# Chunked linear attention ahead of two feed-forward stages: gate logits put before the transposes that turn a unit's rows back, and a weight piece split between two evacuations

## The reference, cut to what matters

```python
# 1: attention with a decaying state, per batch b and head h
state = gamma[h] * state + outer(k[t], v[t])
y[t]  = scale * q[t] @ state                    # x = y as 3072 rows of 512

# 2: each row goes to the one expert with the highest gate logit
logits = x @ w_gate                             # 8 experts
e_idx  = argmax(logits, axis=1)
h      = max(x[mask] @ w1[e], 0)                # 512 -> 1024
out[mask] = gate_w * sigmoid(x @ w_output_gate)[e] * (h @ w2[e])   # 1024 -> 512

# 3: rms norm, then a gated feed-forward layer of width 1536
out = (silu(xn @ w_gate2) * (xn @ w_val)) @ w_out
```

## Time and profile before

| | before |
|---|---|
| time, median of 3 runs | 1107.06 us (1105.83 to 1107.13) |
| the profiled execution's own time | 1104.48 us |
| its span in the profile | 1102.7 us |
| attention stage, from the q transposes of unit 1 to unit 23's `turn_x` | 12.69 to 136.92 us |
| TensorE busy | 1088.8 us (99%) |
| VectorE busy | 442.5 us (40%) |
| ScalarE busy | 378.7 us (34%) |
| GpSimd busy | 177.7 us (16%) |

### The profile page before, as it was taken

The page is one execution under the profiler, slowest core; times in us unless marked ns, Lnnn a source line. Parts: engine busy times, 40 slices in busy tenths (PEclk is TensorE's granted clock), DMA queues, the critical chain, the costliest instruction groups (busy, mean ns, idle before and its releaser), DMA issues.

```text
span 1102.7 us, 20452 instructions
## 1 busy us (share of the span) xinstructions
PE 1088.8 (99%) x6307; PEld 907.5 (82%) x6308; DVE 442.5 (40%) x886; ACT 378.7 (34%) x619; POOL 177.7 (16%) x245
## 2 busy tenths in 40 slices
PE   7999999999999999999999999999999999999998
PEld 6888887888888888887888888888888888888887
DVE  4777766342514425432433323423333243333222
ACT  3555534343525445433224231331133132213112
POOL 2444414222211211000010300210030011001000
PEclk9999999999999999999999999999999999999999
DMA  9999816333435434432101210111021001101001
GB/s 216 254 264 256 232 59 229 123 124 114 124 114 190 164 114 144 155 88 83 58 10 29 77 34 5 38 38 38 0 76 24 14 28 48 38 0 39 1 1 39
DMA packets 114069, 101.53 MB, mean 92 GB/s; under 512 B 81856, under 2 KB 87392, under 8 KB 114016
## 3 DMA queue, kind: packets, MB, share of 16 engines
q1 hardware_dynamic: 98752, 66.07, 22.1%
q0 software_dynamic: 8832, 26.81, 7.7%
q10 hardware_dynamic: 6432, 7.96, 2.1%
HBM read 76.41 MB, written 20.22 MB: 88 GB/s over the span
## 4 chain that ended last, share of the span: by engine, by line
PE 97%; issue 1%; DMA 1%; ACT 0%; POOL 0%; DVE 0%; SPq 0%; POOLq 0%
PE bank L730 15%; PE bank L731 15%; PE bank L732 15%; PE banks L654 14%; PE bank L627 14%; PE banks L730 3%; PE banks L731 3%; PE banks L732 3%; PE bank L538 2%; PE banks L524 2%; PE bank L568 2%; PE bank L576 1%; PE banks L642 1%; PE bank L618 1%; PE banks L517 1%
## 5 line engine op out<-in xcount | busy, mean ns | idle before, releaser
L1409 DVE TENSOR_TENSOR gated<-bank,sig 128x512 f32<-128x512 f32 (+1 forms) x78 | 50.7, 650 | 340.1 <-ACT sig L1022 337.1
L1022 ACT ACTIVATE sig<-bank 128x512 f32<-128x512 f32 x72 | 43.1, 598 | 325.4 <-PE bank L732 315.8
L730 PE MATMUL bank<-xh,w1h 128*128 128x512 f32 x384 | 149.4, 389 | 0.0
L731 PE MATMUL bank<-xl,w1h 128*128 128x512 f32 x384 | 149.4, 389 | 0.0
L732 PE MATMUL bank<-xh,w1l 128*128 128x512 f32 x384 | 149.4, 389 | 0.0
L1031 ACT ACTIVATE hh<-prod 128x512 fp32r<-128x512 f32 (+1 forms) x78 | 46.7, 599 | 109.9 <-DVE prod L1417 105.9
L730 PEld LDWEIGHTS bank<-xh,w1h 128*128 128x128 f32 x384 | 72.1, 188 | 15.0
L732 PEld LDWEIGHTS bank<-xh,w1l 128*128 128x128 f32 x384 | 72.1, 188 | 15.0
L731 PEld LDWEIGHTS bank<-xl,w1h 128*128 128x128 f32 x384 | 72.1, 188 | 14.9
L1176 DVE TENSOR_TENSOR hidl<-bank,hidh 128x512 fp32r<-128x512 f32 x29 | 20.1, 692 | 130.3 <-ACT hidh L881 130.3
L1423 DVE TENSOR_TENSOR hl<-prod,hh 128x512 fp32r<-128x512 f32 (+1 forms) x78 | 50.9, 652 | 51.2 <-ACT hh L1031 48.4
(11 more groups left out here) (243 smaller groups left out, 2139.5 us busy)
## 6 DMA issues: line engine op xcount, KB each, us to landing
stage<-in_moe_w SPq DMA_DIRECT2D x64, 512.0 KB
expert_rows<-tile_o ACTq DMA_DIRECT2D x29, 256.0 KB
q_raw<-in_q SPq DMA_DIRECT2D x24, 256.0 KB
k_raw<-in_k SPq DMA_DIRECT2D x24, 256.0 KB
v_raw<-in_v SPq DMA_DIRECT2D x24, 256.0 KB, 5.0
stage<-stage SPq DMA_DIRECT2D x64, 64.0 KB, 2.0
stage<-in_moe_w_out SPq DMA_DIRECT2D x6, 512.0 KB
stage<-in_moe_w_gate SPq DMA_DIRECT2D x5, 512.0 KB
```

Of the source, the lines that this page charges most:

```text
L730: pe.matmul(out_ap, lh, rh, start=first, stop=False)
L731: pe.matmul(out_ap, lh, rl, start=False, stop=False)
L1022: nc.scalar.activation(sig[:], bank[GV[f % 2][0]][:, :], ACT.Sigmoid).then_inc(s["sig_done"], 1)
L1409: v3.tensor_tensor(gated[:, part], bank[GV[f % 2][0]][:, part], sig[:, part], ALU.mult)\
```

## The change

In TensorE's step `gate_logits(u - 1)` now stands ahead of `turn_x(u - 1)`. In ScalarE's step the split of a weight piece now stands between `evacuate_yT(u - 1)` and `evacuate_x(u - 1)`.

```diff
@@ TensorE, step(u)
                 scores(u)
                 if u:
+                    gate_logits(u - 1)
                     turn_x(u - 1)
-                    gate_logits(u - 1)
@@ ScalarE, step(u)
                 evacuate_turned(u)
                 if u:
                     evacuate_yT(u - 1)
-                    evacuate_x(u - 1)
                 for i in range(PRE_A):
                     if piece_step(i) + 2 == u:
                         split_hi(i % PER, (w1h, w2h)[i // PER % 2], i // RUN * HALF + (i % PER) * PIECE, i // STAGE + 1)
+                if u:
+                    evacuate_x(u - 1)
```

## The result

| | before | after |
|---|---|---|
| median of the runs | 1107.10 us (1105.83 to 1107.26, 4 runs) | 1116.64 us (1115.89 to 1119.04, 4 runs) |
| ratio to before, 95% interval | | 1.0092 [1.0075, 1.0110] |
| the profiled execution's own time | 1104.48 us | 1115.89 us |
| its span | 1102.7 us | 1114.1 us |
| opening of unit 1 to opening of unit 23 | 16.68 to 136.92: 120.24 us | 16.20 to 148.28: 132.08 us |

The change made the kernel 0.92% slower, 9.5 us between the medians and 11.4 us between the two profiled executions. The "opening" of a unit is T of the prediction, where the weight loads behind the scores begin.

A forecast was written before the change was run, and what follows sets the result against it. TensorE, busy for 99% of the span, was taken as the bound. Losses of 10.0 (20 units), 0.40 (unit 12) and 0.88 us (unit 22) sum to 11.3, added to the median 1107.06 for 1118.4 us; range 1115.0 to 1121.7.

The forecast's parts named there:

- The bank wait, 20 x 0.50: K transposes wait for the x_out copy to free turn_x's bank: 0.50 us in each of 20 units, 10.0 us.
- the row behind the last step: Trace row with logits already first; copy started 1.71 us after their first load, giving a loss of 0.65 per unit.
- end of the copy + 0.05 - 1.71: Loss of a unit in us, if positive, from the x_out copy's end counted from T; k loads start undisturbed at 1.67.
- The exchange itself, costed at nothing: TensorE's turn_x, logits and q transposes (0.39, 0.81, 0.47 us) only change places; the exchange by itself adds zero.
- Unit 12 and unit 22: Exceptions: unit 12 loses 0.40, having already lost 0.10 to a late scatter; unit 22 0.88, its logits waiting for slot indices.
- The sum: Whole loss in the attention stage: 10.0 + 0.40 + 0.88 = 11.3 us, giving 1118.4 us.
- The piece: Weight split on ScalarE between the evacuations: 1.05 us, covered by idle time before the copy; no cost.
- The hidden wait: Rival: the k transposes' bank wait stays hidden, the copy ending by T + 1.66; no change, 1107.1 us; chance 0.03.
- the gain from fewer changes of shape: Rival: logits follow the scores without the 0.12 us gap in 23 units, 2.8 us faster, 1104.3; chance 0.02.
- No piece was late: Answers a rival: weight pieces landing late hold the copy back in 12 units, adding 8.0 us, 1126.4; chance 0.06.
- The clock stayed at 1.00: Answers a rival: the clock falls in the run of 12 transposes, adding 26 us, 1144.8; chance 0.02.

The follow-up runs named there:

- own_bank: Changed kernel with turn_x writing unused halves of the outputs' two banks; the outputs, not the k transposes, wait for the x_out copy: 1109.45 us, ratio 1.0025.
- q_ahead: Changed kernel with the next unit's q transposes moved between the logits and turn_x, so the k transposes directly follow turn_x: 1128.22 us, ratio 1.0188.
- q_ahead_old_order: Kernel before with the next unit's q transposes moved ahead of turn_x, leaving only the logits between turn_x and the k transposes: 1113.39 us, ratio 1.0067.
- own_bank_wait_last: Same as own_bank, but the outputs' wait for the x_out copy stands last among their waits, behind that for the state: 1108.08 us, ratio 1.0013.
- three_buffers: Kernel before with a third x_out buffer, so a copy waits for the scatter of three units before instead of two: 1105.41 us, ratio 0.9991.
- logits_only: Kernel before with only the logits moved ahead of turn_x; the weight piece stays behind the copy to x_out: 1117.17 us, ratio 1.0088.
- split_only: Kernel before with only the weight piece's split moved between the two evacuations; turn_x stays ahead of the logits: 1107.36 us, ratio 1.0007.
- own_bank_old_order: Kernel before with turn_x writing unused halves of the outputs' banks, the wait for the copy standing before the outputs: 1105.45 us, ratio 0.9993.
- sum_between: Changed kernel with the state sum moved up between the q and the k transposes: 1118.44 us, ratio 1.0112.

## Why the prediction was right

**The bank wait, 20 x 0.50.** Right in mechanism and size. Forecast: copy ended at T + 2.16, loss 0.50. Measured: T + 2.19 and 0.52. The choice among the rows was right too: the copy starts 0.78 us behind the first load of `turn_x`, nearest to the 0.75 of the k transposes; the row behind the last step, by which the loss came to 0.65, was a poor guide. own_bank shows that the wait for the bank is the cause, and q_ahead and q_ahead_old_order that the rule "end of the copy + 0.05 - 1.71" holds at losses from 0.06 to 0.95.

**The exchange itself, costed at nothing.** That "0.39, 0.81 and 0.47 only change places" isn't quite so: it costs 0.05 us a unit (own_bank_wait_last, 5.67 against 5.62). In the changed kernel that is not to be added: unhindered the k transposes would come at 1.71 instead of 1.67, but they wait until 2.24 in any case.

**Unit 12 and unit 22.** Right: 0.40 forecast and 0.42 measured for unit 12; for the group around unit 22 1.38 forecast (0.50 in unit 21 and 0.88) and 1.42 measured. That unit 12's late copy was the scatter's doing the prediction took from the earlier trace rows, but the four waits there are those of units 7, 17, 19 and 22, and the earlier trace rows puts unit 12's down to TensorE; it is three_buffers, where the loss is gone, that bears it out. "With the copy 0.86 later in the unit, and units longer, the scatter has landed before" failed in two places. Units 5 and 17 still waited for theirs, 0.10 each:

```profile
40.28 0.97 PEld L568 LDWEIGHTS bank<-gates,xT 128*128 128x128 f32 x8
...
41.97 0.60 ACT L816 ACTIVATE x_out<-bank 128x512 f32<-128x512 f32 x1 [2.20 <-DMA x_rows<-x_out,slot_idx]
```

**The sum.** 11.3 forecast; 11.84 in the stage and 11.4 between the profiled executions. The forecast of 1118.4 is 1.8 above the median of 1116.64, since I added the sum to a median 2.6 us above the profiled execution, and the changed kernel's profiled execution lies only 0.75 below its median. A part of that is luck: the profiled execution of the kernel before was faster than all four of its runs, and whether the clock falls behind the attention stage (last section) moves a run by 1.6 us, about as much as the forecast was off.

**The piece.** Covered, as forecast: it starts right behind xT at T - 1.08 (unit 11: T - 0.62) and no split waited for its load. "If it stayed behind the copy it would now reach into the time when qT is due" is true by 0.1 us and worth nothing, as logits_only shows: this half of the change buys nothing.

**The rivals.** The hidden wait and the gain from fewer changes of shape fell with the rows above (the gap of 0.12 behind the scores is there as before, 69.38 to 70.47). No piece was late. The clock stayed at 1.00, 2.4 GHz, through the stage, with 12 transposes in a run and a pause of 0.5 us in it; by the rule of the Trainium skill about transposes and the clock gate ("TensorE: Matmul & The Clock Gate", Part 4) it might have fallen, and here it didn't.

## What to carry to other kernels

Work that stands between a write to a PSUM bank and the next write to the same bank is a cover: before moving it, add up the evacuation from the first load to its signal (1.38 us here) and what is left to cover it (0.47 us of q transposes). A bank wait can be moved to where there is more slack by using free halves of banks that are busy at other times, and it belongs last among the waits ahead of its work (own_bank_wait_last). Where the bounding engine is 99% busy and doesn't wait for a helper, a better place for the helper's work gained nothing (split_only).

## What the runs showed of the hardware that I had not expected

- A wait that had been met 0.16 us before the work was due cost 0.08 us in a unit when another wait stood behind it, and nothing when it stood last (5.75 and 5.67 us).
- A state sum of 16 small matmuls, moved between two groups of transposes, cost 0.30 us more than in its old place, without any wait that the profile shows.
- How late a scatter frees its buffer varies between executions of nearly the same program. The copies that it held up started 5.8 to 6.6 us behind its issue in the kernel before, up to 7.7 in split_only (unit 22) and 7.5 in q_ahead_old_order. In q_ahead none was held up, but there each copy comes 7.5 us or more behind that issue anyway.
- Behind the attention stage the clock falls in some executions. Ahead of the gated layer TensorE is idle for 2.0 us, in all eleven profiles. In six of them the granted clock stays at 1.00 (2.4 GHz); in own_bank_wait_last, own_bank_old_order, q_ahead, q_ahead_old_order and sum_between it then falls to 0.50 (1.2 GHz), while TensorE is busy, and comes back. First own_bank_wait_last, from 0.3 us behind that idle time, then the kernel before at the same place:

```profile
511.70:515.00 3.30, 3.30 (x9) 2.52 (x8) 0.00 (x0) 1.28 (x1) 0.00 (x0) 0.50 0.08 29
```

```profile
509.70:513.00 3.30, 3.30 (x16) 2.70 (x15) 0.00 (x0) 1.28 (x1) 0.00 (x0) 1.00 0.06 20
```

The first 36 products of the gated layer take 9.9 us instead of 8.3, and from the opening of unit 23 to the end pass 967.4 to 968.0 us with the fall and 965.8 to 966.8 without. So 1.6 us of a difference between two executions can come from there, with whichever kernel; in three_buffers the four fastest runs, 1104.3 to 1104.9, are the four with a mean granted clock of 1.000, and the other seven, at 0.998, take 1105.4 to 1106.9.
- TensorE's slow start lasted longer in one execution. In sum_between the 4 loads of the k transposes of unit 1 still took 0.63 us, where they took 0.47 in the kernel before, and unit 1 opened at 19.33 (first the row of sum_between's timeline, then its stretch):

```profile
16.15 0.63 PEld L504 LDWEIGHTS bank<-con,k_s 128*128 128x128 f32 x4
```

```profile
16.00:18.00 2.00, 2.00 (x26) 1.52 (x22) 0.01 (x1) 0.94 (x2) 0.00 (x0) 1.00 1.35 218
```

Some 1.4 us of that late opening is the edit's own: with the state sum ahead of them the k transposes of unit 0 come later, and its scores start at 12.05 instead of 10.68. In the other ten profiles unit 1 opened between 15.63 and 17.34 us, a spread of 1.7. The granted clock reads 1.00 in these stretches, so it doesn't show this slow pace. Opening and clock together are large enough for the spread of the runs, 2.5 us in three_buffers; how much each makes of it was not tested.
